# Shifting all weight buffers by 64 bytes against the columns they meet, in a feed-forward kernel of row-tiled matmul pairs

## What is computed

```python
# x: 4 x 4096 x 192, weight_gen: 4 x 4096 x 8 x 7, w_in: 192 x 2048, w_out: 2048 x 192
w = softmax(weight_gen)                            # over the 7 taps
conv = einsum('bshk,bskhg->bshg', w, x_windows)    # 16384 tokens of 192
h = conv @ w_in
out = (h * (1.0 / (1.0 + exp(-1.702 * h)))) @ w_out
```

## Time and profile before

| | |
|---|---|
| median of 3 runs | 1129.38 us (1128.94 to 1129.43) |
| profiled execution | 1129.01 us, its span 1127.2 us |
| PE, matmuls in flight | 1113.8 us, 99% of the span |
| PE, weight loads | 914.3 us, 81% |
| DVE | 803.6 us, 71% |
| ACT | 620.5 us, 55% |
| DMA | 42.68 MB, mean 38 GB/s |
| granted clock of PE | 1.00 |

### The profile page before, as it was taken

How to read it: one execution, slowest core, us unless ns; L and a number is a source line. 1 busy time by engine, 2 the same in 40 slices (tenths; PEclk the granted TensorE clock), 3 DMA queues, 4 the chain that set the end, 5 groups by cost and what they waited for, 6 DMA issues and landing times.

```text
span 1127.2 us, 21689 instructions
## 1 busy us (share of the span) xinstructions
PE 1113.8 (99%) x9748; PEld 914.3 (81%) x9748; DVE 803.6 (71%) x714; ACT 620.5 (55%) x655; POOL 7.9 (1%) x9
## 2 busy tenths in 40 slices
PE   7999999999999999999999999999999999999998
PEld 4788878888888888888888888888888888888886
DVE  7998988677576866759667596775867757686322
ACT  6676655565554646455464555545556555454543
POOL 2000000000000000000000000000000000000000
PEclk9999999999999999999999999999999999999999
DMA  8601010101001010010100101001010100100000
GB/s 274 218 7 53 15 53 2 39 29 40 29 1 40 29 40 29 1 40 29 40 29 1 65 4 40 29 22 46 1 40 29 40 29 1 40 29 1 29 1 29
DMA packets 8892, 42.68 MB, mean 38 GB/s; under 512 B 1056, under 2 KB 1312, under 8 KB 6496
## 3 DMA queue, kind: packets, MB, share of 16 engines
q1 hardware_dynamic: 8400, 40.51, 10.9%
q0 software_dynamic: 400, 0.79, 0.4%
HBM read 24.77 MB, written 12.58 MB: 33 GB/s over the span
## 4 chain that ended last, share of the span: by engine, by line
PE 94%; DVE 4%; ACT 1%; DMA 0%; issue 0%; ACTq 0%; DVEq 0%; SPq 0%
PE hid L630 45%; PE acc_main L646 30%; PE acc_rest L646 20%; DVE conv L393 1%; DVE gate_lo L548 1%; DVE prod L386 1%; DMA gate<-in_x_first 0%; ACT gate_hi L313 0%; ACT gate L310 0%; DVE hid L469 0%; DVE w L441 0%; DVE prod L411 0%; DVE prod L463 0%; ACT L255 0%; ACT L310 0%
## 5 line engine op out<-in xcount | busy, mean ns | idle before, releaser
L310 ACT ACTIVATE gate<-hid 128x1024 f32<-128x1024 f32 x256 | 263.1, 1028 | 464.6 <-PE hid L630 463.9
L548 DVE TENSOR_TENSOR gate_lo<-gate,gate_hi 128x1024 fp32r<-128x1024 f32 x256 | 311.5, 1221 | 258.0 <-ACT gate_hi L313 258.0
L630 PE MATMUL hid<-xt,w_hi 64*128 64x512 f32 x3072 | 431.8, 387 | 0.0
L630 PEld LDWEIGHTS hid<-xt,w_hi 64*128 64x128 f32 x3072 | 287.4, 184 | 62.7 <-ACT gate_hi L313 2.1
L646 PE MATMUL acc_main<-gate_hi,w 64*128 64x512 f32 x2048 | 315.8, 386 | 0.7 <-DVE gate_lo L548 0.7
L313 ACT ACTIVATE gate_hi<-hid 128x1024 fp32r<-128x1024 f32 x256 | 261.1, 1020 | 0.0
L646 PEld LDWEIGHTS acc_main<-gate_hi,w 64*128 64x128 f32 x2048 | 191.5, 184 | 42.0 <-DVE gate_lo L548 1.7
L630 PE MATMUL hid<-xt,w_lo 64*128 64x512 f32 x1536 | 215.8, 386 | 0.0
L646 PE MATMUL acc_main<-gate_lo,w 64*128 64x512 f32 x1024 | 199.4, 386 | 0.0
L646 PE MATMUL acc_rest<-gate_hi,w 64*128 64x512 f32 x1024 | 199.4, 386 | 0.0
L646 PE MATMUL acc_rest<-gate_lo,w 64*128 64x512 f32 x1024 | 199.4, 386 | 0.0
(11 more groups left out here) (54 smaller groups left out, 228.1 us busy)
## 6 DMA issues: line engine op xcount, KB each, us to landing
xwin<-in_x_runs SPq DMA_DIRECT2D x15, 1056.0 KB, 4.9
out<-outs_main SPq DMA_DIRECT2D x13, 512.0 KB, 2.6
out<-outs_rest SPq DMA_DIRECT2D x13, 256.0 KB, 2.9
taps<-in_tap_runs SPq DMA_DIRECT2D x1, 3136.0 KB, 10.0
taps<-in_w_rows SPq DMA_DIRECT2D x2, 1536.0 KB, 9.8
w_hi<-w_hi SPq DMA_DIRECT2D x2, 768.0 KB, 9.5
w_lo<-w_lo SPq DMA_DIRECT2D x2, 768.0 KB, 7.2
out<-outs_main SPq DMA_DIRECT2D x6, 256.0 KB, 2.1
```

The costliest lines, as they stand in the source:

```text
L310: nc.scalar.activation(gate[:, v % 2, :, :], hid[:, v % 2, :, :], ACT.Gelu_apprx_sigmoid).then_inc(gate_ready, 1)
L548: nc.vector.tensor_tensor(gate_lo[:, v % SLOTS, :, :], gate[:, v % 2, :, :], gate_hi[:, v % SLOTS, :, :], ALU.subtract).then_inc(gate_lo_r ...
L630: last = nc.tensor.matmul(hid[:, v % 2, h, :], w[rows, k if j else slice_of(h, k), q, f], xt[rows, j % 2, part, k, :], start=(i == 0), sto ...
```

## The change

A helper `sb_on` allocates a buffer that is `HALF` = 64 elements (256 bytes) longer than what it is to hold, and gives out the part that begins `ON` = 16 elements (64 bytes) after its start. `w1_hi`, `w1_lo` and `w2` are made with it; everything else, the order of instructions included, is as before. Each begins 64 bytes later against the grid of 256 bytes, and all other tensors keep their places on that grid.

```diff
+ON = 16
...
-        w1_hi = sb("w1_hi", [P, SLICES, 2, FH], F32R)
-        w1_lo = sb("w1_lo", [P, SLICES, 2, FH], F32R)
-
-        w2 = sb("w2", [P, CH, 2 * D], F32R)
+        def sb_on(name, pattern, n, **sizes):
+
+            return sb(name, [P, n + HALF], F32R)[:, ON:ON + n].rearrange(pattern, **sizes)
+
+
+        w1_hi = sb_on("w1_hi", "p (k q f) -> p k q f", SLICES * 2 * FH, k=SLICES, q=2)
+        w1_lo = sb_on("w1_lo", "p (k q f) -> p k q f", SLICES * 2 * FH, k=SLICES, q=2)
+
+        w2 = sb_on("w2", "p (c d) -> p c d", CH * 2 * D, c=CH)
```

## The result

The changed kernel takes 1159.22 us (median of 4 runs, 1159.04 to 1159.29); beside it the kernel before takes 1129.31. The ratio is 1.0266, 95% interval 1.0253 to 1.0279: 30 us slower. The forecast was 1129.4 us and the range ended at 1148. Its direction was that of rival C, with a price even above the one given there.

What follows compares the result with a forecast made beforehand. PE's matmul pairs were taken to bound the kernel, 4,864 at 226.7 ns. Pitch, load and writer terms summed 0 + 0 + 0 = 0 us, so 1,129.4 us was forecast, range 1,092 to 1,148 us.

Steps and rivals of the forecast that it cites:

- rival C: Shift puts weight load and column stream in each other's way: up to 232 ns a pair, +26 us, 1,155.2 us; chance 0.17.
- The bound of -51 us in the sum: Lower bound on the change from the pair pitch, beside +26 us, around a forecast sum of 0 us.
- rival B: Shift frees the column stream: 216 ns a pair and 52 us less at full size, 26 us at half; chance 0.34.
- rival D: Weight load becomes the bound through its new start, past 226.7 ns a pair: from 1,135 us up; chance 0.03.
- the writers: Roundings and remainders writing or reading weights 64 bytes off, two ahead of the first pairs: 0 taken, at most 0.35 us.
- the copies: Four copies doubling the w1 buffers: first read at 188 us, hidden by more than 120 us even if doubled.
- Does the load disturb the stream?: Step on PE's pairs: streams partly without a load weren't faster, so the 13.4 ns has nothing to do with addresses; no change.
- late load: Weight load starting 0.06 to 0.19 us into a stream, before 84.50 and 117.04 us and in the stream from 17.98.
- A: No change, the forecast: 1,129.4 us, argued from late loads and a steady pitch despite ACT and DVE traffic; chance 0.46.
- The restarts at 232 ns: After a late load, five pairs from 84.50 to 85.66 us take 232 ns each; some phase sets the pitch within a few nanoseconds.
- 13.4 unexplained ns: Pair pitch of 226.7 ns above the 213.3 ns of 512 columns at 2.4 GHz; 65 us over 4,864 pairs.
- 3 ns from the transposes: Transposes 109 ns apart, 2.7 ns above twice 53.3, read as some 3 ns extra per load and stream; as floor, 216 ns.

Runs made afterwards that it cites:

- experiment 3: Padded kernel with weights 0 or 64 bytes past the columns, 17 of 19 pairs loading 64 of 128 weight columns: 1142.95 and 1154.31 us.
- Experiments 1 and 2: First: see experiment 1. Second: changed kernel with only `ON` varied, weights 16 to 320 bytes past columns (padding doubled for 320): 1129.17 to 1159.37 us.
- experiment 1: Changed kernel with weights back at 0, padding kept: 1129.22 us; columns moved to 64 too: 1129.01; weights at 0, columns at 64: 1139.31.

## Why the prediction was wrong

**What held.** PE's pace alone was in question, and the span moved by the change of pitch times 4,864 pairs less 2 us of stalls that vanished. (The bound of -51 us in the sum is the 52 us of rival B: 10.7 x 4.864.) The load stayed far from being the bound (rival D), the writers cost 6 ns, the copies were hidden. The buffers did share a start modulo 256, and the change did what it says.

**The step that failed** is "Does the load disturb the stream?", with its conclusion: "That speaks for a cost of starting a pair that has nothing to do with addresses, and for no change." The reading of the rows was sound: streams with a late load were no shorter (226, 227 and 226 ns by the trace's starts to the nanosecond), and the short loads of experiment 3 point the same way: less overlap doesn't buy a faster pair. The inference was not. From "the pitch doesn't go with how long both reads overlap" it went to "the pitch doesn't depend on where the two reads stand", and only the first was in the rows. Experiments 1 and 2 show that the second is false: the same instructions take 544 cycles or 560 by the distance alone.

**The argument for A failed likewise.** That ACT and DVE at changing places don't change PE's pace held in both kernels from 200 to 1100 us, and says nothing on PE's own two reads.

**The sign that was weighed too low.** The restarts at 232 ns showed that the same pairs can run slower, and the prediction set it down under C as "the present phase may be a good one that a shift can lose". In its outcome that is what came: of ten places tried, seven run at 233.3 ns, and 0 is one of two at 226.7. C had 0.17. Its price of 26 us at most was the restarts' mean made lasting; measured were 32.4 us in pairs, and 30 in the whole. That the two are so close may be luck: a restart goes 236, 228, 233, 231 ns and is then back at 226, the changed kernel stays at 233 or 234, and no run shows that they are the same thing. The range ended at 1,148, between half of C's price and the whole, and 11 us short.

**Rival B** rested on 13.4 unexplained ns. By the prediction's count of one column a cycle, 32 cycles a pair remain at the best distances, and no distance tried takes any of them away. Its floor, 3 ns from the transposes, was weaker than it looked: they follow one another after 109 ns, and so do loads when nothing holds them up, 0.11 us in the earlier trace rows. The transposes may have been going at the pace of their loads, and then they say nothing of what a stream costs beyond its columns.

The Trainium skill, "TensorE: Matmul & The Clock Gate", section "Step-by-step: what each phase is for", says that loading the next weights through a port of its own takes no read bandwidth from the running matmul. The measurement decides against using that as "places don't matter": with 184 ns for a load at either place, the distance alone moves the pitch from 226.7 to 233.3 ns. That the stream's bandwidth is what is lost is not shown either.

**What stays open** is the mechanism. The runs exclude the padding, the absolute place, the other half of the partitions and the load as the bound, and, as far as experiment 3 can tell, the amount of overlap. They leave something that depends on the distance and on what stands beside a pair (short loads, short streams, pairs at another distance), and that lands, where all pairs are alike, on multiples of 16 cycles over one pair or over three. The prediction named one way to be wrong, that the start of a stream is the only place where the two reads meet; the runs neither show it nor exclude it. Why 0 and 240 are good, 192 half good and 16 bad is not explained by anything here. Four-byte shifts, distances between columns of successive streams, and loads with other strides were not tried.

## What to carry to other kernels

Where a kernel is bound by a stream of load and matmul pairs, the start of the weights against the start of the moving columns, modulo 256 bytes, is a parameter like any other: 3% lay in it here. A buffer inserted between the two can change it by accident, if its size isn't a multiple of 256 bytes; one in front of both moves them together, which cost nothing in experiment 1. Measure the pitch over hundreds of pairs (starts of units in the chain, or the count in a long stage) and look at what fraction of places is as good as the present one before moving off it. And a row that shows that two things don't compete for time doesn't show that they are independent of each other's place.

## What the runs showed of the hardware that wasn't expected

- A pair of 64-row matmuls of 512 f32r columns never ran steadily under 544 cycles (226.7 ns) in any kernel here; at one column a cycle, which no run here shows by itself, they would be 512. Leaving out 128 of the columns made a pair at distance 0 shorter by 51 ns (226.7 to 175.9).
- At 16 bytes the pitch is 233.2 ns and at 240, which is 16 on the other side, 226.6: the dependence isn't symmetric about 0.
- One matmul on half the partitions takes as long as two side by side on both halves: 1128.90 us with 5,756 matmuls, 1128.73 beside it with 9,748.
- Shorter weight loads, with half of the result's rows left out, made the kernel slower at distance 0 (1142.95 us for 1129.22) while they made it faster at 64 (1154.31 for 1159.22).
- At 192 bytes three pairs together take 1,648 cycles, a multiple of 16, and no single one does (549.33 on average, 228.89 ns).
- Pairs at distance 0 that are mixed with pairs at distance 64 take 230 ns in place of 226.7 (2.07 us for 9).
